# Moving a float32 attention, MoE and FFN kernel's SBUF tiles: matmul weights and inputs to multiples of 1024 bytes, intermediates 704 bytes behind one

## What is computed

```
x   = attention(q, k, v)     # B=8, H=8, S=576, D=64; k and v mean-pooled by 8 keys
x   = moe(x)                 # 4608 tokens, 512 wide, 8 experts of 1024, top 2
out = (h - tanh(h)) @ w_out  # h = x @ w_in, 512 -> 2048 -> 512
# an expert: out[mask] += weight * (relu(x[mask] @ w1[e]) @ w2[e])
```

## Time and profile before

| | |
|---|---|
| time, median of 3 runs | 2073.27 us (2071.35 to 2075.6) |
| the profiled execution | 2070.45 us |
| its span, first to last instruction | 2068.7 us |
| mean granted clock of TensorE | 0.973 |
| attention and routing | 0 to 341 us |
| experts | 356 to 1238 us |
| FFN | 1256 us to the end |

### The profile page before, as it was taken

The page is one execution under the profiler, slowest core; times in us unless marked ns, Lnnn a source line. Parts: engine busy times, 40 slices in busy tenths (PEclk is TensorE's granted clock), DMA queues, the critical chain, the costliest instruction groups (busy, mean ns, idle before and its releaser), DMA issues.

```text
span 2068.7 us, 36878 instructions
## 1 busy us (share of the span) xinstructions
PE 1942.2 (94%) x13280; PEld 1744.3 (84%) x13281; DVE 1055.1 (51%) x2002; ACT 836.8 (40%) x1776; POOL 562.8 (27%) x527
## 2 busy tenths in 40 slices
PE   5888882999999999999999996999999999999999
PEld 5677671989899999999998986889999889999888
DVE  6778864313131313132131316766777766777765
ACT  4566562323232323232232324444444444444444
POOL 3354535112121112112212122222222222322222
PEclk9999995999999999999999998999999999999999
DMA  7545323314131313212131312001000001100000
GB/s 210 135 126 147 102 61 108 126 41 138 46 132 51 122 42 115 66 63 105 56 122 53 129 46 97 32 30 61 30 30 30 30 30 51 40 30 30 30 30 21
DMA packets 79077, 152.34 MB, mean 74 GB/s; under 512 B 12768, under 2 KB 37472, under 8 KB 76224
## 3 DMA queue, kind: packets, MB, share of 16 engines
q1 hardware_dynamic: 62720, 108.42, 16.7%
q0 software_dynamic: 16320, 43.45, 6.3%
HBM read 111.51 MB, written 40.33 MB: 73 GB/s over the span
## 4 chain that ended last, share of the span: by engine, by line
PE 86%; DVE 7%; issue 3%; DMA 2%; POOL 1%; ACT 1%; DVEq 0%; SPq 0%; POOLq 0%; ACTq 0%
PE banks L715 13%; PE banks L714 13%; PE banks L713 13%; PE banks L704 12%; PE banks L705 12%; PE banks L706 12%; PE banks L694 3%; PE banks L601 2%; PE banks L620 2%; PE banks L580 1%; PE banks L589 1%; DVE kp L1022 1%; DMA v_raw<-in_v 1%; DVE mx L1033 1%; DMA k_raw<-in_k 1%
## 5 line engine op out<-in xcount | busy, mean ns | idle before, releaser
L704 PE MATMUL banks<-x_hi,w_hi 128*128 128x256 f32 x2304 | 639.3, 277 | 5.1 <-DVE x_lo L1232 4.1
L705 PE MATMUL banks<-x_lo,w_hi 128*128 128x256 f32 x2304 | 638.6, 277 | 0.0
L706 PE MATMUL banks<-x_hi,w_lo 128*128 128x256 f32 x2304 | 638.6, 277 | 0.0
L713 PE MATMUL banks<-w_hi,h_hi 128*128 128x512 f32 x1184 | 467.1, 395 | 3.0 <-DVE h_lo L1256 3.0
L715 PE MATMUL banks<-w_hi,h_lo 128*128 128x512 f32 x1184 | 466.1, 394 | 0.0
L714 PE MATMUL banks<-w_lo,h_hi 128*128 128x512 f32 x1184 | 463.0, 391 | 0.0
L704 PEld LDWEIGHTS banks<-x_hi,w_hi 128*128 128x128 f32 x2304 | 435.1, 189 | 8.1 <-DVE x_lo L1232 4.9
L705 PEld LDWEIGHTS banks<-x_lo,w_hi 128*128 128x128 f32 x2304 | 435.2, 189 | 2.5
L706 PEld LDWEIGHTS banks<-x_hi,w_lo 128*128 128x128 f32 x2304 | 435.0, 189 | 0.0
L542 POOL TENSOR_SCALAR large<-u_sq 128x512 uint8<-128x512 f32 x144 | 222.6, 1546 | 585.5 <-ACT u_sq L971 317.6
L1239 DVE SCALAR_TENSOR_TENSOR h_lo<-banks,h_hi 128x512 fp32r<-128x512 f32 x144 | 99.6, 692 | 379.7 <-ACT h_hi L922 379.7
(11 more groups left out here) (141 smaller groups left out, 2223.7 us busy)
## 6 DMA issues: line engine op xcount, KB each, us to landing
w_raw<-in_moe_w SPq DMA_DIRECT2D x32, 1024.0 KB, 5.0
y<-y_rows SPq DMA_DIRECT2D x18, 1024.0 KB, 5.0
k_raw<-in_k SPq DMA_DIRECT2D x32, 288.0 KB
q_sb<-in_q SPq DMA_DIRECT2D x32, 288.0 KB, 10.5
v_raw<-in_v SPq DMA_DIRECT2D x8, 1152.0 KB
x_rows<-x_sb SPq DMA_DIRECT2D x32, 288.0 KB, 3.6
out_x<-y_sb SPq DMA_DIRECT2D x36, 256.0 KB, 2.1
w_raw<-in_moe_w_in SPq DMA_DIRECT2D x4, 1024.0 KB, 4.9
```

What stands on the lines that cost most here:

```text
L704: pe.matmul(part, hi, x_hi[:, c, :], start=(c == 0), stop=False)
L705: pe.matmul(part, hi, x_lo[:, c, :], start=False, stop=False)
L706: mm = pe.matmul(part, lo, x_hi[:, c, :], start=False, stop=(c == NC - 1))
L713: pe.matmul(p_y[m][:, :], hi, w_hi[par][:, o:o + DM], start=(j == 0), stop=False)
```

## The change

Three kinds of things are moved. `c_w[0]`, `idx_g` and `idx_s` and a spacer of 32 bytes go ahead of the weights, which moves the weights, `w_raw`, and all attention tiles by 256 bytes. The spacer of 320 bytes ahead of `y2` goes, so `y2`, `x_hi` and `x_lo` come right behind the weights. `large`, `c_w[1]` and a spacer of 32 bytes go between `x_lo` and `h_hi`.

```diff
         blocks = sb("blocks", [1, 4 * E], i32)
+        c_w = [sb("c_w0", [128, TC])]
+        idx_g = sb("idx_g", [128, SUB], i32)
+        idx_s = sb("idx_s", [128, SUB], i32)
+        sb("spacer0", [128, 8])
         w_hi = [sb("w_hi0", [128, WE], f32r)]
...
         w_lo.append(sb("w_lo1", [128, WE], f32r))
-        c_w = [sb(f"c_w{i}", [128, TC]) for i in range(2)]
-        idx_g = sb("idx_g", [128, SUB], i32)
-        idx_s = sb("idx_s", [128, SUB], i32)
-        sb("spacer", [128, 80])
         y2 = sb("y2", [128, SUB, 2 * DM])
         xg = y2[:, :, 0:DM]
         x_hi = sb("x_hi", [128, NC, NB], f32r)
         x_lo = sb("x_lo", [128, NC, NB], f32r)
+        large = sb("large", [128, 2 * NB], mybir.dt.uint8)
+        c_w.append(sb("c_w1", [128, TC]))
+        sb("spacer1", [128, 8])
         h_hi = sb("h_hi", [128, FT2, NB], f32r)
...
         th = sb("th", [128, 2 * NB])
-        large = sb("large", [128, 2 * NB], mybir.dt.uint8)
```

## The result

The changed kernel takes 2115.1 us (median of 4 runs, 2110.89 to 2118.26) beside 2072.31 us for the kernel before: a ratio of 1.0203, with a 95% interval of 1.0178 to 1.0229. It is slower, by some 43 us; the interval leaves open whether the loss is just under or over 2%. The forecast was no change, and the range to 2084 did not reach it.

The account below looks back on a forecast made before the run. TensorE, which never waits from 356 us on but at the gaps, was taken as the bound. The terms, four zeros and -0.2 on 2070.45, gave 2070.2 us against the profiled execution, likeliest median 2072.8, range 2057 to 2084.

Parts of the forecast that it names:

- The bound: Experts and FFN: TensorE never waits from 356 us on outside two gaps, so its pace from start to start matters.
- third rival: `up`: x and weights collide at distance 0, adding 1.1 to 2.2 ns a matmul, 2081 to 2088 us; chance 0.20.
- Weights against `h`: `down`: both move by 256 bytes, distance stays 704; 0 taken, gain at most 56.5 us, loss at most 8.0.
- `x` against the weights: `up`: distance goes from 704 to 0; 0 taken, gain at most 45.6 us, loss at most 15.2 us.
- second rival: TensorE matmuls: the whole excess, 102 us, depends on place; a third to all goes, 2039 to 1971 us; chance 0.12.
- first rival: `down`: its 2.2 ns tail goes as weights start at a multiple of 1024, 8.0 us less, 2065 us; chance 0.24.
- The other engines and the transfers: ScalarE copies: place at most 2%, 0 taken; transfers into `y2`: 0 gain, at most 0.1 us each.

Follow-up runs that it names:

- e16: Changed kernel with x and y2 alone put back to 704 bytes behind the weights, as in e1; 2155.58 us against 2156.3 for the kernel before, ratio 0.9998.
- e4: Tiles placed with weights at 768 within 1024, x 256 bytes and h 512 bytes behind them; 2193.38 us beside 2157.46 for the kernel before.
- e3: Against the changed kernel, weights at 768 within 1024, x 128 bytes behind them, h at distance 0; 2197.18 us beside 2157.46 for the kernel before.
- e9: Only tiles moved: x 192 bytes and h 256 bytes behind the weights; 2098.32 us against 2070.19 for the kernel before, ratio 1.0144.
- e7: Only tiles moved: x 224 bytes and h 32 bytes behind the weights; 2122.44 us beside 2071.24 for the kernel before.
- e5: Only tiles moved: x 64 bytes and h 160 bytes behind the weights; 2119.37 us beside 2071.24 for the kernel before.
- e10: Changed kernel, no tile moved, loaded pieces shifted inside their tiles by a different amount per group; 2105.83 us beside 2070.19 for the kernel before.
- e14: Kernel before, with down loading its h pieces 52 elements further down, at distance 240 within 256; 2169.21 us beside 2157.33 for the kernel before.
- e11: Kernel before, with down loading its h pieces 48 elements further down, at distance 0 within 256; 2180.07 us beside 2157.33 for the kernel before.
- e1: Changed kernel with x and y2 alone put back to 704 bytes behind the weights; 2156.49 us beside 2157.46 for the kernel before.

## Why the prediction was wrong

**The bound: right.** TensorE stayed the bound, no wait came or went, and its pace from start to start was the thing to read. The last paragraph named the third rival's mark, `up` over 113.9 ns with `down` unchanged, and that is what the profile shows.

**Weights against `h`: right in the value.** 0 was taken, and e16 has 0.9998 for the absolute move of both. `down` is at 228.9 before and after. The second argument for it was no argument: that `down` steps through pieces of `h` 512 bytes apart without a change of pace could not show that place is without effect, since 512 and 0 give the same pace (e4).

**`x` against the weights: the step that failed.** I took 0, and it is 6.7 ns a matmul on the other side, 46 us by count and 40.9 in the trace. The argument was that distances of 704 and of 192 both occur without a change of pace. They are 192 and 192 within 256: the one value was seen many times, and no second one. The other argument, that 6.6 and 7.8 ns are nearly alike at two places of the moving operand, compared absolute places, 448 and 768; the distance was 192 in both pairs. The rows did not cover a distance of 0, as the text itself said, and should have carried little weight in the value taken, and the range should have been wider on the side of the loss.

**The third rival: right that the distance counts, wrong in size, and half right in the mechanism.** It took a distance of 0 for a collision and the others for free. The table says otherwise: 96, 128 and 160 give `up` the same 120.0 ns, and every distance tried but 192 costs 3.4 ns or more. The kernel before lay at the one good distance, and leaving it was the loss, not arriving at 0. Its price was 1.1 to 2.2 ns a matmul, from `down`'s excess over `up`; 6.7 ns was measured, as much again as all of the excess that `up` had (120.0 - 106.7 = 13.3 against 6.6). The bound of the loss came from a row at one distance, and a collision that no row shows was priced by what is left where there is least of it. The symmetric bound was at hand: the whole 6.6 ns once more, 45.6 us, stood there as a bound of the gain only. Its chance, 0.20, was low for that reason too: the trace showed an excess over the columns' own time and gave it no owner.

**The second rival: not borne out.** No distance that was tried brought `up` under 113.3 ns, where the mark was 112, or 512 columns under 226.7. Those 6.7 ns over the 106.7 of `up`, and 13.3 over 213.3, stay without an owner.

**The first rival: half right.** The 2.2 ns of `down` do depend on place, and go at distance 0 (e3, e4, e9). But not by pieces of 1024: the weights lie at a multiple in the changed kernel, and `down` has them still.

**The other engines and the transfers: right**, as far as the runs tell. ScalarE's copies, compare:

```profile
L906 ACT ACTIVATE w_hi<-w_raw 128x512 fp32r<-128x512 f32 x160 | 89.4, 621 | 15.7 <-DMA w_raw<-in_moe_w 15.7
...
L980 ACT ACTIVATE h_hi<-g 128x512 fp32r<-128x512 f32 x144 | 91.2, 633 | 61.4 <-DVE g L1307 47.5
```

621 and 633 ns as before. Within 256 bytes nothing moved there, for `g32` and `h_hi` lie at 192 before and after. But they lie at 0 in e3 and e4, at 32 in e7, at 160 in e9 and at 224 in e5, and the copy took 633 or 634 ns in all of them: the 12 ns are not the place. The transfers TensorE waits for took 4.36 and 4.76 us instead of 4.29 and 4.84, so the start at a multiple of 256 did not show in them. The 0.2 us that the sum took off for it are not borne out.

**Not settled:** the attention ended 6.7 us later in the profiled execution, and 4 to 8 us later in e5 to e10. The move of its tiles cannot be all of it, since e16, with the same move by 256 bytes, has a ratio of 0.9998, and e7, with these tiles where they lay before, still ended the attention 5.8 us later. The spread of that stage is no full answer either: in e9 the four runs take 28 us more by the medians while the part behind the attention takes 20.4 more. No run took it apart.

## What to carry to other kernels

When TensorE is the bound and both operands are four-byte float32r, compare the step from start to start with the step at half clock divided by two: part of an excess that nothing in the trace owns may be the distance between the stream and the load beside it, within 256 bytes. Test it by moving the loaded piece inside its tile, a different shift for each group of matmuls, and one run gives eight distances, as they come out in that order. Then try the best distances together, since one phase's pace can depend on the one before it; and before steps of a pattern count as evidence of insensitivity, reduce them by the period that is in question.

## What the runs showed of the hardware

- The pace of float32r matmuls depends on where the streaming operand and the next one's loaded piece lie to each other. At full clock 256 columns took 113.3 to 120.0 ns and 512 columns 226.7 to 234.3, by the distance of the two addresses within 256 bytes and, at one distance, by what ran ahead. The best of both, 113.3 and 226.7, are 1.06 times the 106.7 and 213.3 ns that the half-clock step gives. Why the distance counts is not shown. The Trainium skill (TensorE: Matmul & The Clock Gate, Step-by-step: what each phase is for) says that loading the next weights takes no SBUF read bandwidth from the running matmul. These runs do not fit that, for this type: up to 6.7 ns of a matmul of 256 columns hang on the place of what is loaded beside it.
- Where the group at 192 bytes had 113.3 ns, the groups at 188 and 196 had 118.2 and 119.7, each behind another group (e10).
- At one distance the pace can be locked to either of two values, 113.3 or 117.8 ns, for a whole stretch of 96 or 192 matmuls (e14). The pieces that the `down` ahead loads can choose it (e11), a stand of 0.63 us in the midst of an `up` went with a change from 117.8 to 113.3 (e9), and one kernel had either pace in the same `up` in two executions (e1, e16).
- While ScalarE, VectorE and GpSimd read and wrote SBUF beside it, `up`'s settled pace did not move by a tenth of a ns over 54 `up`s, in the kernel before and in the one after.
